# Padding tensors of the on-chip memory, so that the operands of the matmuls begin at multiples of 2 KB, and one of them 64 bytes behind

## The chip, the cores and the metric

The kernel runs on 1 core of one Trainium2 chip. The metric is the device time of one execution in microseconds (us). A core has TensorE (PE, the matmuls; the load of its stationary operand is listed apart as PEld), VectorE (DVE), ScalarE (ACT), GpSimd (POOL) and SyncE (SP, which here only issues DMAs). Operands lie in the on-chip memory, 128 partitions side by side; a tensor has the same byte offset in each partition, and this case is about that offset. TensorE writes to a memory of its own, the PSUM (here the tensors `H`, `YP`, `OP`).

## The reference

A channel attention over 6016 tokens of 256 channels, and then two feed-forward networks (FFNs), each from 256 to 2048 and back:

```python
qn = q / (np.linalg.norm(q, axis=1, keepdims=True) + 1e-06)     # q, k, v: (1, 6016, 256)
kn = k / (np.linalg.norm(k, axis=1, keepdims=True) + 1e-06)
s = kn.transpose(0, 2, 1) @ qn / tau                             # 256 x 256
a = softmax(s);  x = v @ a
h = x @ w_in1                                                    # 6016 x 2048
g = (a0 + a1*h + a2*h**2 + a3*h**3) / (1 + |b0|*|h| + |b1|*h**2 + 1e-6)
x = g @ w_out1                                                   # 6016 x 256
h = x @ w_in2                                                    # 6016 x 2048
g = h * clip(h + 3, 0, 6) / 6
out = g @ w_out2                                                 # 6016 x 256
```

## The kernel before, in words

**Stages.** `q` and `k` are loaded piece by piece (`qk`) and multiplied into a 256x256 sum in `OP` (line 471, in fp32). The softmax follows, and the attention matrix is folded into the first FFN's up-projection (`fold`, line 511), so that the rest of the kernel is two FFNs on `v`. The tokens are then worked off in 12 blocks: a first one of 384 tokens, and 11 of 512. The hidden 2048 are cut into 16 chunks of 128.

**Split products.** Each FFN product is made of three matmuls in fp32r (fp32 numbers that TensorE takes at one pass): both factors are split into a high and a low part (`_hi`, `_lo`), and `split_product` (lines 438 to 440) issues hi by hi, hi by lo and lo by hi into the same sum.

**The order on TensorE.** It is written out by hand in `step` (a loop over blocks `t`, with its chunks `j`). In each chunk TensorE issues four groups, 30 matmuls in all:

- `up2`: 6 matmuls of 512 columns. The moving operand is `yT_hi` or `yT_lo` (half c of the channels, 2 KB of each partition), the stationary one a slice of 128 columns (512 bytes) of `wu2_hi` or `wu2_lo`. The sum is in `H`.
- `down2`: 12 matmuls of 256 columns (lines 594, 596, 598). Here the gate is the stationary operand: four slices of 128 tokens (512 bytes) of `g2_hi` or `g2_lo`, and `wd2_hi` or `wd2_lo` moves (1 KB a chunk).
- `up1`: 6 matmuls of 512 columns. `vT_hi` or `vT_lo` moves, slices of `wf_hi`, `wf_lo` are stationary. The sum is in `H`.
- `down1`: 6 matmuls of 512 columns. The first FFN's gate, `g1_hi` or `g1_lo` (2 KB a chunk, four buffers), moves; slices of `wd1_hi`, `wd1_lo` are stationary. The sum is in `YP`.

The profile's names join some tensors: `g_hi` is `g1_hi` under `YP` and `g2_hi` under `OP`; `wd_hi`, `wu_hi` likewise.

Between the groups the gates are worked out from PSUM by ACT, DVE and POOL (lines 692 to 725, 889 to 937, 392 to 406), each held to TensorE by semaphores. `T`, `SQ`, `AB`, `Y` and `R` hold values on the way.

**Where the tensors lie.** They are placed one behind the other in the order in which the code makes them (`sb(name, shape, dt)`), each at the next free byte of the partition, rounded up to 32. There is some reserved space first, which ends 1152 bytes past a multiple of 2 KB. `wf`, `wd1`, `wd2`, `wu2` take 16 KB each, `vT` 4 KB each, so that all of these begin 1152 bytes past a multiple of 2 KB. Then come `ident`, `ones` (512 bytes each) and small tensors, then `v_blocks` (4 KB), `coef_row` and `o_tok` (4 KB); those small ones take 1344 bytes in all. From `o_tok` on (`w_raw_a` and `qk` in the attention's stage; `yT`, `R`, `g2`, `T`, `SQ`, `AB`, `Y`, `g1` in the same bytes later) everything begins 448 bytes past a multiple of 2 KB.

Of the kernel before, what the change touches and what calls it, by code (L numbers as in the profile page):

```python
# [20 lines left out]
fp32 = mybir.dt.float32  # L21
# [5 lines left out]
P = 128  # L27


def attention_ffn_ffn(nc, q, k, v, tau, w_in1, w_out1, a, b, w_in2, w_out2, out):  # L30
# [63 lines left out]
    with ctx:  # L94
        def sb(name, shape, dt, stack=ctx):
            return stack.enter_context(nc.sbuf_tensor(name, shape, dt))
# [2 lines left out]
            return ctx.enter_context(nc.semaphore(name))  # L99


        wf_hi, wf_lo = (sb(f"wf_{x}", [P, CT, F], f32r) for x in ("hi", "lo"))
        wd1_hi, wd2_hi = (sb(f"{x}_hi", [P, J, C], f32r) for x in ("wd1", "wd2"))
        wu2_hi = sb("wu2_hi", [P, CT, F], f32r)
# [15 lines left out]
        absb = sb("absb", [P, 2], fp32)  # L120
        root_b1 = sb("root_b1", [P, 1], fp32)[:]
        small = sb("small", [P, 48], fp32)

        v_blocks = sb("v_blocks", [P, CT, W], fp32)
        v_tok = v_blocks[:].rearrange("p h w -> p (h w)").rearrange("p (i c) -> p i c", c=C)
# [14 lines left out]

        yT_hi, yT_lo = (sb(f"yT_{x}", [P, CT, W], f32r) for x in ("hi", "lo"))
        R = sb("R", [P, 2, W], fp32)
        g2_hi, g2_lo = (sb(f"g2_{x}", [P, 4, W], f32r) for x in ("hi", "lo"))

        T = sb("T", [P, 2, W], fp32)
        SQ = sb("SQ", [P, 4, W], fp32)
# [67 lines left out]
        def back(blk, j, n):  # L214

            blk, j = blk + (j - n) // J, (j - n) % J
            return None if isinstance(blk, int) and blk < 0 else (blk, j)

        def wait_chunk(engine, semaphore, at):
            if at is not None:  # L220
                engine.wait_ge(semaphore, count(*at))
# [31 lines left out]
        def h2(blk, j):  # L253
            return H[:, 2 + j % 2, 0:width(blk)]
# [103 lines left out]
        def _(pool):  # L358
# [42 lines left out]
            def g2_split(blk, j):  # L401
                w = width(blk)
                if last_chunk(blk, j):
                    return
                wait_chunk(pool, g2_hi_done, (blk, j))
                nc.gpsimd.tensor_tensor(g2_lo[:, j % 4, 0:w], R[:, j % 2, 0:w], g2_hi[:, j % 4, 0:w].bitcast(fp32),  # L406
                                        ALU.subtract).then_inc(g2_lo_done, 1)
# [213 lines left out]
        def _(act):  # L621
# [93 lines left out]
            def c1(blk, j):  # L715
                w = width(blk)
                wait_chunk(act, u2_done, (blk, j))
                wait_chunk(act, g2_lo_done, back(blk, j, 2))
                nc.scalar.activation(R[:, j % 2, 0:w], h2(blk, j), ACT.Relu, bias=3.0).then_inc(r_done, 1)  # L719

            def c2(blk, j):
                w = width(blk)
                wait_chunk(act, g2_done, (blk, j))
                wait_chunk(act, d2_done, back(blk, j, 4))
                nc.scalar.activation(g2_hi[:, j % 4, 0:w], R[:, j % 2, 0:w], ACT.Copy).then_inc(g2_hi_done, 1)  # L725

# [68 lines left out]
        def _(dve):  # L795
# [126 lines left out]
            def gate2(blk, j):  # L922
                w = width(blk)
                wait_chunk(dve, r_done, (blk, j))
                nc.vector.scalar_tensor_tensor(R[:, j % 2, 0:w], R[:, j % 2, 0:w], 6.0, h2(blk, j),  # L925
                                               ALU.min, ALU.mult).then_inc(g2_done, 1)
                if last_chunk(blk, j):
                    wait_chunk(dve, g2_hi_done, (blk, j))
                    wait_chunk(dve, d2_done, back(blk, j, 4))
                    nc.vector.tensor_tensor(g2_lo[:, j % 4, 0:w], R[:, j % 2, 0:w],  # L930
                                            g2_hi[:, j % 4, 0:w].bitcast(fp32), ALU.subtract).then_inc(last_lo_done, 1)
# [57 lines left out]
```

## Time and profile before

| | |
|---|---|
| median of 3 runs | 1139.7 us (1139.54 to 1140.29) |
| the profiled execution | 1139.15 us, of it 1137.3 us span |
| PE busy | 1112.0 us, 98% of the span, 6012 matmuls |
| PEld busy | 961.3 us, 85% |
| DVE, ACT, POOL busy | 890.6 us (78%), 879.3 us (77%), 781.5 us (69%) |
| granted clock of TensorE | 0.995 of full |
| waits of PE on others | the longest group 7.8 us |

The span is the time from the first to the last recorded instruction. A matmul's busy time is longer than its share of the engine: matmuls overlap, and the next one starts while the one before is still under way. The pace is read from the distance between starts.

### The profile page before, as it was taken

How to read it: one execution, taken by the hardware profiler on the slowest of the kernel's cores; microseconds unless marked ns; L12 is line 12 of the kernel's file. 1: busy time of each engine (PE TensorE's matmuls, PEld its weight loads, DVE VectorE, ACT ScalarE, POOL GpSimd, SP SyncE). 2: the span in 40 equal slices, each digit the busy share in tenths (PEclk: the TensorE clock that was granted, in tenths of full speed). 3: DMA queues.
4: the chain of work that ended last, by engine and by line, in shares of the span. 5: the costliest groups of instructions: out<-in, count | busy, mean ns of one | idle time of the engine just before them, and what ended most of it. 6: DMA issues, size and time to landing. Idle time of an engine off the chain costs nothing.

```text
span 1137.3 us, 17913 instructions
## 1 busy us (share of the span) xinstructions
PE 1112.0 (98%) x6012; PEld 961.3 (85%) x6012; DVE 890.6 (78%) x1264; ACT 879.3 (77%) x1479; POOL 781.5 (69%) x625
## 2 busy tenths in 40 slices
PE   9988799999999999999999999999999999999998
PEld 8877588888888888888888888888888888888887
DVE  6699999887887887887887787787787787787722
ACT  6698888877877877877787787787787787787643
POOL 0278888776776776676676676677677677666643
PEclk9999899999999999999999999999999999999999
DMA  9931010010010010010010010010001000000000
GB/s 343 305 116 20 1 19 1 15 19 2 20 19 1 20 19 2 2 36 1 1 38 1 2 38 1 1 31 8 2 19 19 1 20 1 1 20 1 1 19 19
DMA packets 65729, 34.21 MB, mean 30 GB/s; under 512 B 47718, under 2 KB 58982, under 8 KB 65638
## 3 DMA queue, kind: packets, MB, share of 16 engines
q1 hardware_dynamic: 65072, 32.52, 10.1%
q8 instruction: 52, 0.85, 0.3%
q10 hardware_dynamic: 566, 0.52, 0.1%
q14 instruction: 39, 0.32, 0.1%
HBM read 26.87 MB, written 6.16 MB: 29 GB/s over the span
## 4 chain that ended last, share of the span: by engine, by line
PE 91%; DVE 5%; ACT 1%; issue 1%; DMA 0%; POOL 0%; SPq 0%; DVEq 0%; ACTq 0%
PE H L438 15%; PE H L440 14%; PE H L439 14%; PE OP L594 8%; PE OP L598 7%; PE OP L596 7%; PE YP L438 7%; PE YP L440 7%; PE YP L439 7%; PE OP L471 3%; DVE SQ L911 1%; DVE H L896 1%; DVE g_hi L904 1%; DVE T L889 1%; DMA qk<-in_k 0%
## 5 line engine op out<-in xcount | busy, mean ns | idle before, releaser
L392 POOL TENSOR_TENSOR SQ<-SQ,AB 128x512 f32<-128x512 f32 (+1 forms) x192 | 247.7, 1290 | 271.9 <-ACT SQ L694 271.6
L406 POOL TENSOR_TENSOR g_lo<-R,g_hi 128x512 fp32r<-128x512 f32 (+1 forms) x191 | 243.7, 1276 | 28.2 <-ACT g_hi L725 28.2
L398 POOL TENSOR_TENSOR g_lo<-SQ,Y 128x512 fp32r<-128x512 f32 (+1 forms) x192 | 244.2, 1272 | 6.2 <-DVE SQ L919 6.2
L692 ACT ACTIVATE AB<-H,absb 128x512 f32<-128x512 f32 (+1 forms) x192 | 130.6, 680 | 143.7 <-PE H L440 142.9
L594 PE MATMUL OP<-wd_hi,g_hi 128*128 128x256 f32 x748 | 208.1, 278 | 0.0
L598 PE MATMUL OP<-wd_hi,g_lo 128*128 128x256 f32 x748 | 207.8, 278 | 0.0
L596 PE MATMUL OP<-wd_lo,g_hi 128*128 128x256 f32 x748 | 207.8, 278 | 0.0
L889 DVE TENSOR_TENSOR T<-T,H 128x512 f32<-128x512 f32 (+1 forms) x192 | 129.4, 674 | 97.3 <-ACT T L700 97.3
L904 DVE SCALAR_TENSOR_TENSOR g_hi<-H,coef,Y 128x512 fp32r<-128x512 f32 (+1 forms) x192 | 141.7, 738 | 65.9 <-ACT Y L713 64.6
L438 PE MATMUL H<-vT_hi,wf_hi 128*128 128x512 f32 (+1 forms) x384 | 152.2, 396 | 13.6 <-DVE wf_lo L876 7.8
L911 DVE SCALAR_TENSOR_TENSOR SQ<-SQ,g_hi 128x512 f32<-128x512 f32 (+1 forms) x192 | 156.2, 814 | 6.6
L719 ACT ACTIVATE R<-H 128x512 f32<-128x512 f32 (+1 forms) x192 | 113.6, 591 | 57.1 <-PE H L440 56.4
L925 DVE SCALAR_TENSOR_TENSOR R<-R,H 128x512 f32<-128x512 f32 (+1 forms) x192 | 128.1, 667 | 36.9 <-ACT R L719 36.9
L438 PE MATMUL YP<-g_hi,wd_hi 128*128 128x512 f32 (+1 forms) x384 | 151.6, 395 | 4.9 <-POOL g_lo L398 3.3
L439 PE MATMUL H<-vT_lo,wf_hi 128*128 128x512 f32 (+1 forms) x384 | 150.8, 393 | 0.0
L438 PE MATMUL H<-yT_hi,wu_hi 128*128 128x512 f32 (+1 forms) x384 | 149.6, 390 | 0.8 <-issue 0.6
L440 PE MATMUL H<-yT_hi,wu_lo 128*128 128x512 f32 (+1 forms) x384 | 149.7, 390 | 0.0
L440 PE MATMUL YP<-g_hi,wd_lo 128*128 128x512 f32 (+1 forms) x384 | 149.1, 388 | 0.0
L439 PE MATMUL YP<-g_lo,wd_hi 128*128 128x512 f32 (+1 forms) x384 | 149.0, 388 | 0.0
L440 PE MATMUL H<-vT_hi,wf_lo 128*128 128x512 f32 (+1 forms) x384 | 148.7, 387 | 0.0
L896 DVE SCALAR_TENSOR_TENSOR H<-T,coef,H 128x512 f32<-128x512 f32 (+1 forms) x192 | 143.0, 745 | 6.8
L700 ACT ACTIVATE T<-H,coef 128x512 f32<-128x512 f32 (+1 forms) x192 | 147.8, 770 | 0.0
(98 smaller groups left out, 2208.1 us busy)
## 6 DMA issues: line engine op xcount, KB each, us to landing
qk<-in_q SPq DMA_DIRECT2D x22, 256.0 KB, 5.7
qk<-in_k SPq DMA_DIRECT2D x22, 256.0 KB, 6.9
v_blocks<-in_v SPq DMA_DIRECT2D x88, 64.0 KB, 2.3
out<-o_tok SPq DMA_DIRECT2D x10, 512.0 KB, 3.0
wd_raw<-in_moe_w_out SPq DMA_DIRECT2D x8, 512.0 KB, 9.3
w_raw_a<-in_moe_w_in SPq DMA_DIRECT2D x2, 1024.0 KB, 11.1
wu_raw<-in_moe_w_in SPq DMA_DIRECT2D x4, 512.0 KB, 6.3
qk<-in_q SPq DMA_DIRECT2D x3, 128.0 KB, 2.7
```

What stands on the lines that cost most here:

```text
L392: nc.gpsimd.tensor_tensor(SQ[:, j % 4, 0:w], SQ[:, j % 4, 0:w], AB[:, j % 2, 0:w], ALU.add)\
L398: nc.gpsimd.tensor_tensor(g1_lo[:, j % 4, 0:w], SQ[:, j % 4, 0:w], Y[:, j % 2, 0:w], ALU.mult)\
L406: nc.gpsimd.tensor_tensor(g2_lo[:, j % 4, 0:w], R[:, j % 2, 0:w], g2_hi[:, j % 4, 0:w].bitcast(fp32), ALU.subtract).then_inc(g2_lo_done, 1)
L438: nc.tensor.matmul(psum, w_hi, x_hi, start=first, stop=False)
L439: nc.tensor.matmul(psum, w_hi, x_lo, start=False, stop=False)
L440: return nc.tensor.matmul(psum, w_lo, x_hi, start=False, stop=last)
L594: nc.tensor.matmul(psum, g2_hi[:, j % 4, at], wd2_hi[:, j, :], start=first, stop=False, skip_group_check=True)
L596: nc.tensor.matmul(psum, g2_hi[:, j % 4, at], wd2_lo[:, j, :], start=False, stop=False, skip_group_check=True)
L598: done = nc.tensor.matmul(psum, g2_lo[:, j % 4, at], wd2_hi[:, j, :], start=False, stop=last, skip_group_check=True)
L896: nc.vector.scalar_tensor_tensor(h, T[:, j % 2, 0:w], A1, h, ALU.add, ALU.mult).then_inc(t3_done, 1)
L904: nc.vector.scalar_tensor_tensor(g1_hi[:, j % 4, 0:w], h1(blk, j), A0, Y[:, j % 2, 0:w], ALU.add, ALU.mult).then_inc(g1_hi_done, 1)
L911: nc.vector.scalar_tensor_tensor(SQ[:, j % 4, 0:w], SQ[:, j % 4, 0:w], Q_CONST, g1_hi[:, j % 4, 0:w].bitcast(fp32), ALU.add, ALU.mult).the ...
```

## The change

Four tensors are made that nothing reads or writes. They push what is made behind them to other offsets; no instruction is added, removed or moved in the order.

```diff
+        sb("up_to_2_kb", [P, 224], fp32)
         wf_hi, wf_lo = (sb(f"wf_{x}", [P, CT, F], f32r) for x in ("hi", "lo"))
...
         small = sb("small", [P, 48], fp32)
+        sb("up_to_4_kb", [P, 176], fp32)
 
         v_blocks = sb("v_blocks", [P, CT, W], fp32)
...
         R = sb("R", [P, 2, W], fp32)
+        sb("g2_offset", [P, 16], fp32)
         g2_hi, g2_lo = (sb(f"g2_{x}", [P, 4, W], f32r) for x in ("hi", "lo"))
+        sb("up_to_next_2_kb", [P, 496], fp32)
 
         T = sb("T", [P, 2, W], fp32)
```

The pads take 896, 704, 64 and 1984 bytes of each partition, 3648 in all. After it `wf`, `wd1`, `wd2`, `wu2` and `vT` begin at a multiple of 2 KB (1152 + 896 = 2048), `o_tok`, `w_raw_a`, `qk`, `yT` and `R` too (448 + 896 + 704 = 2048), `g2_hi` and `g2_lo` 64 bytes behind one, and `T`, `SQ`, `AB`, `Y`, `g1` at one again.

## Rows read from the trace of the kernel before

**Rows 1.** The page: busy time by engine, and busy tenths of 40 slices.
```profile
PE 1112.0 (98%) x6012; PEld 961.3 (85%) x6012; DVE 890.6 (78%) x1264; ACT 879.3 (77%) x1479; POOL 781.5 (69%) x625
PE   9988799999999999999999999999999999999998
PEclk9999899999999999999999999999999999999999
```
**Rows 2.** Waits of PE: who waited for whom, total us, times, longest.
```profile
PE H L438 <- DVE wf_lo L876: 7.8, 7, 2.3
PE H L438 <- DVE SQ L919: 5.7, 2, 5.1
```
**Rows 3.** Stretches: length, then busy us (instructions) by engine, clock, DMA, GB/s.
```profile
0.00:60.00 60.00, 56.45 (x271) 48.74 (x272) 39.03 (x55) 41.62 (x56) 11.86 (x13) 1.00 0.98 325
60.00:150.00 90.00, 72.75 (x353) 63.60 (x352) 84.20 (x135) 77.56 (x150) 73.97 (x65) 0.94 0.11 31
150.00:1137.00 987.00, 982.78 (x5392) 849.00 (x5391) 767.42 (x1076) 760.11 (x1275) 695.67 (x549) 1.00 0.05 12
300.00:1070.00 770.00, 769.41 (x4170) 661.31 (x4169) 617.20 (x866) 606.93 (x1014) 549.78 (x433) 1.00 0.05 12
```
**Rows 4.** PE in order of time, one chunk: start us, length us, matmul.
```profile
499.89 0.39 PE L438 MATMUL H<-yT_hi,wu_hi 128*128 128x512 f32 x1
...
501.04 0.40 PE L440 MATMUL H<-yT_hi,wu_lo 128*128 128x512 f32 x1
501.27 0.28 PE L594 MATMUL OP<-wd_hi,g_hi 128*128 128x256 f32 x1
...
501.97 0.28 PE L594 MATMUL OP<-wd_hi,g_hi 128*128 128x256 f32 x1
...
502.31 0.28 PE L594 MATMUL OP<-wd_hi,g_hi 128*128 128x256 f32 x1
...
502.65 0.40 PE L438 MATMUL H<-vT_hi,wf_hi 128*128 128x512 f32 x1
...
504.04 0.40 PE L438 MATMUL YP<-g_hi,wd_hi 128*128 128x512 f32 x1
...
504.74 0.39 PE L438 MATMUL YP<-g_hi,wd_hi 128*128 128x512 f32 x1
...
505.43 0.39 PE L438 MATMUL H<-yT_hi,wu_hi 128*128 128x512 f32 x1
```
**Rows 5.** PE in order of time, the last block (up2 and down2 alone).
```profile
1100.31 0.39 PE L438 MATMUL H<-yT_hi,wu_hi 128*128 128x512 f32 x1
...
1101.68 0.28 PE L594 MATMUL OP<-wd_hi,g_hi 128*128 128x256 f32 x1
```
**Rows 6.** The chain that ended last, in the attention: start, us, what.
```profile
22.98 20.72 PE OP L471 x96
```
**Rows 7.** PE and PEld groups of 300 to 1070 us: busy us, mean ns.
```profile
L439 PE MATMUL H<-vT_lo,wf_hi 128*128 128x512 f32 x278 | 109.9, 395 | 0.0
L440 PE MATMUL H<-yT_hi,wu_lo 128*128 128x512 f32 x278 | 109.7, 395 | 0.0
L440 PE MATMUL H<-vT_hi,wf_lo 128*128 128x512 f32 x278 | 108.2, 389 | 0.0
L439 PE MATMUL H<-yT_lo,wu_hi 128*128 128x512 f32 x278 | 107.9, 388 | 0.0
L439 PEld LDWEIGHTS H<-vT_lo,wf_hi 128*128 128x128 f32 x278 | 52.2, 188 | 5.6
```
**Rows 8.** The costliest DVE group, 128x512, whole span.
```profile
L911 DVE SCALAR_TENSOR_TENSOR SQ<-SQ,g_hi 128x512 f32<-128x512 f32 x176 | 143.1, 813 | 6.1
```

## The prediction

> **What bounds the kernel now.** I read the busy times first. PE is busy 98% of the span, at full clock, while DVE, ACT and POOL stand at 78, 77 and 69% [rows 1]. That alone proves little, because overlapping matmuls flatter PE, so the second look is at its waits: the two longest groups are 7.8 and 5.7 us in 1137.3 [rows 2], and both belong to the first stretch. The third is the table of stretches. From 60 to 150 us PE is busy 72.75 of 90 us, and DVE 84.20: there, while the fold and the first block run, DVE sets the pace. From 150 us on PE is busy 982.78 of 987 us, and from 300 to 1070 us 769.41 of 770, against 617.20 for DVE [rows 3]. So for 987 us nothing but the rate at which TensorE takes matmuls matters, and a change that touches no instruction can act on the time through that rate alone.
>
> **That rate.** The stretch of 770 us holds 4170 matmuls, and a chunk has 30, so it holds 139 chunks, 770 / 139 = 5.540 us each [rows 3]. One chunk in order of time splits it [rows 4]: `up2` from 499.89 to 501.27 is 1.38 us for 6 matmuls, 230 ns each; `down2` from 501.27 to 502.65 is 1.38 us for 12, 115 ns each; `up1` to 504.04 and `down1` to 505.43 are 1.39 us each, 232 ns a matmul. The sum is 5.54 us. Within the groups the pace isn't even. The second half of `down2`, 501.97 to 502.65, has 6 matmuls in 0.68 us, 113 ns each, against 117 ns in its first half [rows 4]. In the last block, where `up2` and `down2` alternate alone, the 6 long matmuls from 1100.31 to 1101.68 take 1.37 us, 228.3 ns each [rows 5].
>
> What could these be at best? In the attention 96 fp32 matmuls take 20.72 us, 215.8 ns each [rows 6]; they have 256 columns and evidently take two passes a column, so that they are as long as 512 columns of one pass. A long FFN matmul takes 230 to 232, 14 to 16 ns more. In a chunk 18 x 15 = 270 ns, and over the span some 50 us, are lost against the attention's pace, in a place where no engine waits. The excess differs between groups that are built alike: the matmuls with `vT_lo` moving are recorded with a mean of 395 ns and those with `yT_lo` with 388, `yT_hi` over `wu_lo` with 395 and `vT_hi` over `wf_lo` with 389 [rows 7]. `up1` and `up2` have the same instructions, the same sizes and the same sum tensor; they differ in the offsets of their operands and in the group ahead. So offsets may well matter at the level of 7 ns in a matmul (3%), and that is the only door this change has.
>
> The Trainium skill speaks against it. The page "SBUF — State Buffer", section "Who interferes with whom", gives TensorE two independent read ports, for the moving operand and for the weights, and says that it waits for nobody; "Operand start alignment" there calls the start address a matter of what is legal, not of speed. The page "TensorE: Matmul & The Clock Gate", section "Back-to-back issue gap", has N/2.4 + 2.5 ns, which is 215.8 ns for 512 columns. By this rule the sum of the change would be nothing. The attention's 215.8 ns agree with it [rows 6]; the FFNs' 230 to 232 ns don't [rows 4], so something acts there that the rule doesn't hold.
>
> **The change part by part.** No instruction goes or comes, no wait changes, and every wait is on the same semaphore as before.
>
> 1. *`wf`, `wd1`, `wd2`, `wu2`, `vT` from 1152 bytes past a multiple of 2 KB to 0; `yT`, `g1`, `w_raw_a`, `qk` from 448 to 0.* Two things change: the place in a 2 KB row, and the place of moving against stationary operand. The first I price low: slices of the gate `g2` begin at 448, 960, 1472 and 1984 bytes, so only the fourth crosses a multiple of 2 KB, and the third and fourth slices' matmuls from 501.97 to 502.31 and from 502.31 to 502.65 take 0.34 us each [rows 4]. A crossing costs nothing there. The second is the candidate: now `up1` has moving and stationary operands at like offsets, `up2` and `down1` at unlike ones (448 against 1152), `down2` likewise, and the reads of each matmul run beside the load of the next one's weights, so that at a change of group the relation changes too. The slow first halves of `down2` (117 against 113) stand just behind such a change.
> 2. *`g2` 64 bytes behind.* It acts on the weight loads of `down2`, and on the last matmul of `up2`, beside which the first of these loads runs. That one is the slowest of its group: 501.04 to 501.27, recorded with 0.40 us against 0.39 for the first [rows 4]; there both offsets are 448 today, thus alike.
> 3. *`T`, `SQ`, `AB`, `Y`, `R`, `v_blocks`, `o_tok`.* Reads and writes of DVE, ACT, POOL and the DMAs move. The nearest price is the costliest DVE instruction, 813 ns [rows 8]; if alignment took or gave 2% of 84.20 us of DVE in the stretch that DVE sets [rows 3], it would be 1.7 us either way. From 150 us on PE's bound covers it: DVE would have to grow by 770 / 617.20, 25%, before it showed. I take 0.
>
> **The sum.** For the unknown new pace I take the settled one that the trace already has: 228.3 ns for the long matmuls [rows 5] and 113.3 for the short ones [rows 4], since after the change all groups but `down2` share one relation of offsets, and `down2` avoids the equal one. A chunk is then 18 x 228.3 + 12 x 113.3 = 4109 + 1360 = 5469 ns, 71 less than 5540. Chunks in the stretch that PE sets: 987 / 5.54 = 178. The gain is 178 x 0.071 = 12.6 us. The profiled execution took 1139.15 us; less 12.6 that is 1126.6, and as it lies 0.55 us under the median of the runs, the forecast is 1127 us. The bounds of this term: at best the long ones come to the attention's 215.8 ns and the short stay, 18 x 215.8 + 1360 = 5244 ns, 296 less, -52.7 us; at worst every long one takes 240 ns (the slowest matmul of `up2` is recorded with 0.40 us where the first has 0.39, so 10 ns over the mean of 230) and every short one 117 [rows 4]: 4320 + 1404 = 5724 ns, 184 more, +32.8 us. I stay near the settled pace because it is the one that the same instructions already show.
>
> **The rivals.**
>
> *A. The full loss goes.* If the 15 ns are reads of moving and stationary operand that collide because of their starts, and like starts end that, the time is 1139.7 - 52.7 = 1087 us. For it: the attention's matmuls, with `qk` as both operands and thus like starts, have no excess [rows 6]. Against it: `up1` has like starts already and is no faster than the others [rows 4]; the attention reads only half as many columns in that time. DVE would then need 617.20 / 139 = 4.44 us of a chunk of 5.24, so it would not take over. Chance 12%.
>
> *B. Nothing, the change doesn't do what it says for the time.* The excess belongs to the matmuls of one pass a column and the order of groups, not to starts: the uncrossed and the crossing slice are alike, and the four groups lie within 0.01 us although their offsets differ [rows 4]. Time 1139.7 us. This is also where the rule of the Trainium skill's page "SBUF — State Buffer", section "Who interferes with whom", leads: reads that never wait for each other can't be helped by other starts. Chance 17%.
>
> *C. Slower: the like start is the dear one.* `up1`, alike today, shows 395 ns for `vT_lo` where `up2`, unlike, shows 388 for `yT_lo` [rows 7], and the slowest matmul of `up2` is the one beside which an alike load runs. If 12 long ones of `up2` and `down1` each take on 3 to 4 ns, half of that difference, it is 12 x 3.5 = 42 ns a chunk and 7.5 us in all: 1147 us. It decides from the point where what the gate's 64 bytes give back (at most 12 x 2 ns in `down2`) is less than that. Chance 23%.
>
> **How the numbers follow.** The forecast, faster by about 1%, has 48%, A 12%, B 17%, C 23%. A difference of 0.2% (2.3 us) is about what can be told from none. Faster: 48 + 12 = 60%; within 0.2%: 17%; slower: 23%. The likeliest case's own range is 1112 to 1137. The range for 8 in 10 reaches up into C, to 1149, and down between forecast and A, to 1100, leaving out most of A and the far end of C.
>
> **What would show it.** In the profile after, 139 chunks' worth of matmuls (4170) should take some 760 us in place of 770 in the middle stretch; the short ones should start 113 ns apart from the first on, the long ones 228. `yT_lo` and `vT_lo` matmuls should show the same mean. If `down2` alone changes, the 64 bytes are what acts; if the three long groups change alike, the common start. PE's busy share and waits should stay as they are. I am wrong if the distance between starts is unchanged (B), or if the long ones stand at 232 or more (C); and if the time moves while the pace of the middle stretch doesn't, the cause is in the first 150 us and part 3 was priced too low.

## The result, and the profile after

The kernel after takes 1136.69 us (median of 8 runs, 1136.19 to 1137.52) against 1139.64 us for the kernel before in the same comparison. The ratio is 0.9974, with a 95% interval of [0.9963, 0.9985]: faster by 0.26%, some 3 us. The forecast was 12.6 us. In the experiments below, one execution of the kernel before (1502 us) and one of x1 (2244 us) stand far from all others of their kernel, and the ratios leave them out.

The page of the kernel after, and its stretches (length, then busy us and instructions of PE, PEld, DVE, ACT, POOL, then clock, DMA share and GB/s), answer to [rows 1] and [rows 3]:

```profile
PE 1111.2 (98%) x6012; PEld 968.4 (85%) x6012; DVE 889.9 (78%) x1264; ACT 878.8 (77%) x1479; POOL 781.0 (69%) x625
```

```profile
0.00:60.00 60.00, 56.78 (x269) 48.95 (x270) 38.61 (x55) 41.46 (x55) 11.46 (x13) 1.00 0.95 316
60.00:150.00 90.00, 73.29 (x352) 64.02 (x351) 84.24 (x135) 77.48 (x151) 73.94 (x64) 0.94 0.13 37
300.00:1070.00 770.00, 769.24 (x4178) 667.73 (x4178) 617.59 (x868) 608.10 (x1017) 550.59 (x434) 1.00 0.05 12
```

Nothing but the pace has moved. PE is as busy as before, DVE takes 84.24 us of the second stretch against 84.20, and the two longest waits of PE are again 7.8 and 5.7 us:

```profile
PE H L444 <- DVE wf_lo L882: 7.8, 7, 2.3
PE H L444 <- DVE SQ L925: 5.7, 2, 5.1
```

In the same 770 us PE starts 4178 matmuls in place of 4170, so that a chunk takes 770 / (4178 / 30) = 5.529 us, 0.011 less (a rough count, since a few matmuls are missing from a trace). One chunk in order of time (start, length in us) shows where; it answers to [rows 4], with line 444 for 438 and 600 for 594:

```profile
505.06 0.39 PE L444 MATMUL H<-yT_hi,wu_hi 128*128 128x512 f32 x1
...
506.42 0.28 PE L600 MATMUL OP<-wd_hi,g_hi 128*128 128x256 f32 x1
...
507.12 0.28 PE L600 MATMUL OP<-wd_hi,g_hi 128*128 128x256 f32 x1
...
507.83 0.40 PE L444 MATMUL H<-vT_hi,wf_hi 128*128 128x512 f32 x1
...
509.22 0.39 PE L444 MATMUL YP<-g_hi,wd_hi 128*128 128x512 f32 x1
...
510.58 0.39 PE L444 MATMUL H<-yT_hi,wu_hi 128*128 128x512 f32 x1
```

`up2` has gone from 1.38 to 1.36 us and `down1` from 1.39 to 1.36; `up1` stays at 1.39; and `down2` has gone up, from 1.38 to 1.41. Its second half, 507.12 to 507.83, takes 0.71 us, 118 ns a matmul, where it took 113. The groups of 300 to 1070 us (busy us, mean ns) say it over all chunks and answer to [rows 7]:

```profile
L600 PE MATMUL OP<-wd_hi,g_hi 128*128 128x256 f32 x557 | 156.5, 281 | 0.0
L445 PE MATMUL H<-vT_lo,wf_hi 128*128 128x512 f32 x278 | 109.9, 395 | 0.0
L445 PE MATMUL H<-yT_lo,wu_hi 128*128 128x512 f32 x280 | 108.9, 389 | 0.0
L446 PE MATMUL H<-yT_hi,wu_lo 128*128 128x512 f32 x280 | 108.8, 389 | 0.0
L446 PE MATMUL YP<-g_hi,wd_lo 128*128 128x512 f32 x279 | 108.5, 389 | 0.0
```

All forms of `up2` and `down1` are now at 389 ns (390 for one), where `up2` over `wu_lo` stood at 395. A matmul's recorded length is its distance to the next start plus some 162 ns, so 389 is a start every 227 ns and 395 one every 233. `vT_lo` stays at 395.

### The profile page after: what moved, and what is told of

Read it like the earlier page. It is cut to its first block, busy times and chain, and to the rows that moved or that the text cites. A ratio compares the mean times of both kernels' runs of the same rounds, so it can differ in the third digit from the quotient of the medians.

```text
span 1135.7 us, 17913 instructions
## 1 busy us (share of the span) xinstructions
PE 1111.2 (98%) x6012; PEld 968.4 (85%) x6012; DVE 889.9 (78%) x1264; ACT 878.8 (77%) x1479; POOL 781.0 (69%) x625
## 4 chain that ended last, share of the span: by engine, by line
PE 91%; DVE 5%; ACT 1%; issue 1%; DMA 0%; POOL 0%; SPq 0%; DVEq 0%; ACTq 0%
PE H L444 15%; PE H L445 14%; PE H L446 14%; PE OP L604 8%; PE OP L600 8%; PE OP L602 8%; PE YP L445 7%; PE YP L446 7%; PE YP L444 7%; PE OP L477 3%; DVE SQ L917 1%; DVE H L902 1%; DVE g_hi L910 1%; DVE T L895 1%; DMA qk<-in_k 0%
## 5 line engine op out<-in xcount | busy, mean ns | idle before, releaser
L602 PEld LDWEIGHTS OP<-wd_lo,g_hi 128*128 128x128 f32 x748 | 142.7, 191 | 6.5
```

Source lines behind the costliest of these rows:

```text
L602: nc.tensor.matmul(psum, g2_hi[:, j % 4, at], wd2_lo[:, j, :], start=False, stop=False, skip_group_check=True)
```

## The experiments

All of them move tensors and nothing else. I give an offset as a distance: the start of the stationary operand less that of the moving one, counted within 256 bytes (why 256, x7 and x8 show). In the trace the first weights of a group are loaded beside the last matmul of the group ahead, so each change of group has a distance too. The table has two of them: `g2` less `yT` at the entry to `down2`, and `wf` less `wd2` at its exit. The way into `down1` (`wd1` less `vT`) is 0 in all kernels. The way into `up2` (`wu2` less `g1`) is 192 in before and x1, 128 in x6, 64 in x7 and x8, and 0 in all the others. The table gives each group's time as the mean over the chunks of 300 to 1070 us, in ns, from the starts of all matmuls in the trace (a few with a wait behind them left out; each cell is rounded by itself). The last two columns are the chunk's difference to before times 178, the chunks in the stretch that PE sets, and the measured difference of the medians.

| kernel | distances up2, down2, up1, down1 | entry, exit | up2 | down2 | up1 | down1 | chunk | x 178, us | measured, us |
|---|---|---|---|---|---|---|---|---|---|
| before | 192, 64, 0, 192 | 0, 0 | 1380 | 1377 | 1387 | 1390 | 5534 | | |
| after | 0, 64, 0, 0 | 64, 0 | 1359 | 1413 | 1387 | 1360 | 5520 | -2.5 | -2.95 |
| x1 | as before | 0, 0 | 1380 | 1377 | 1387 | 1390 | 5534 | 0 | +0.1 |
| x2 | as after | 64, 0 | 1359 | 1413 | 1388 | 1360 | 5520 | -2.5 | -2.8 |
| x3 | 0, 0, 0, 0 | 0, 0 | 1360 | 1432 | 1388 | 1360 | 5540 | +1.1 | +1.2 |
| x4 | 0, 192, 0, 0 | 192, 0 | 1359 | 1411 | 1370 | 1360 | 5500 | -6.1 | -5.4 |
| x5 | 0, 64, 0, 0 | 64, 0 | 1359 | 1413 | 1388 | 1360 | 5520 | -2.5 | -3.3 |
| x6 | 192, 64, 0, 128 | 0, 0 | 1392 | 1377 | 1387 | 1392 | 5547 | +2.3 | +0.6 |
| x7 | 0, 0, 0, 64 | 0, 0 | 1380 | 1432 | 1388 | 1400 | 5600 | +11.7 | +11.1 |
| x8 | 128, 128, 0, 64 | 0, 0 | 1403 | 1423 | 1387 | 1400 | 5613 | +14.1 | +13.2 |
| x9 | 0, 64, 0, 0 | 0, 64 | 1360 | 1413 | 1360 | 1360 | 5493 | -7.3 | -7.8 |
| x10 | 192, 64, 0, 0 | 0, 0 | 1397 | 1377 | 1387 | 1360 | 5520 | -2.5 | -2.9 |
| x11 | 0, 32, 0, 0 | 32, 0 | 1368 | 1418 | 1395 | 1372 | 5553 | +3.6 | +3.8 |
| x12 | 192, 64, 0, 0 | 192, 64 | 1390 | 1410 | 1360 | 1360 | 5520 | -2.5 | -2.6 |
| x13 | 0, 192, 0, 0 | 0, 192 | 1360 | 1417 | 1392 | 1364 | 5533 | -0.2 | -0.3 |

The sum over a chunk accounts for the time of every one of them within 1.7 us (x6, one run), most within 0.6. x6, x7, x8 and x11 are one run each beside the kernel before.

**x1 and x2: the place in the row, or the distance?** x1 keeps the first pad alone, x2 all but the first:

```diff
 x1
+        sb("up_to_2_kb", [P, 224], fp32)
 x2
+        sb("up_to_4_kb", [P, 176], fp32)
+        sb("g2_offset", [P, 16], fp32)
+        sb("up_to_next_2_kb", [P, 496], fp32)
```

> Of the four pads only the first (896 bytes) stands: every tensor of the FFNs moves by the same amount, wf, wd1, wd2, wu2 and vT to a multiple of 2 KB, yT, g1, g2 and the rest from 448 to 1344 past one, so no offset of one operand against another changes. Theory R (what counts is where the stationary operand begins against the moving one): every group keeps its pace, up2 1.38, down2 1.38, up1 and down1 1.39 us a chunk (5.54), time as before, 1139.6 us within 1.5. Theory M (what counts is the place of an operand in its 2 KB row): up1 has both operands at multiples of 2 KB in the kernel after and is no faster there (1.39 us), but wd1 and wu2 as stationary operands would carry a part of what up2 and down1 gained (0.02 and 0.03 us of a chunk), time 1133 to 1137 us.

> The first pad is taken away and the other three stand: wf, wd1, wd2, wu2, vT, yT and g1 all begin 1152 bytes past a multiple of 2 KB, g2 1216 past one. No operand but for those is at a multiple of 2 KB, but the offsets against each other are those of the kernel after. Theory R: paces as after, up2 and down1 1.36 us, down2 1.41, up1 1.39, time 1136.7 us within 1.5. Theory M: paces as before, 1.38, 1.39, 1.38, 1.39, time 1139.6.

x1: 1139.83 us, ratio 1.0002 [0.9992, 1.0013]. x2: 1136.94 us, 0.9976 [0.9966, 0.9986]. The groups of 300 to 1070 us, first of x1 and then of x2:

```profile
L597 PE MATMUL OP<-wd_hi,g_hi 128*128 128x256 f32 x556 | 154.4, 278 | 0.0
L443 PE MATMUL H<-yT_hi,wu_lo 128*128 128x512 f32 x278 | 109.7, 395 | 0.0
```

```profile
L599 PE MATMUL OP<-wd_hi,g_hi 128*128 128x256 f32 x559 | 157.1, 281 | 0.0
L445 PE MATMUL H<-yT_hi,wu_lo 128*128 128x512 f32 x280 | 108.8, 389 | 0.0
```

x1 has `wf`, `wd1`, `wd2`, `wu2` and `vT` at a multiple of 2 KB, and its lengths are those of before. x2 has no FFN operand at one (1152 and 1216 bytes past), and its lengths are those of after. The multiple of 2 KB does nothing that can be told; the offsets against each other carry the whole change. Theory M falls and R stands.

**x3, x4, x5: where g2 begins.** In the kernel after `g2` is moved to 0, 192 and 320 bytes behind (x5 also makes its pads up to 512 bytes only, not 2 KB):

```diff
 x3
-        sb("g2_offset", [P, 16], fp32)
-        sb("up_to_next_2_kb", [P, 496], fp32)
 x4
-        sb("g2_offset", [P, 16], fp32)
-        sb("up_to_next_2_kb", [P, 496], fp32)
+        sb("g2_offset", [P, 48], fp32)
+        sb("up_to_next_2_kb", [P, 464], fp32)
 x5
-        sb("up_to_2_kb", [P, 224], fp32)
+        sb("up_to_2_kb", [P, 96], fp32)
-        sb("up_to_4_kb", [P, 176], fp32)
+        sb("up_to_4_kb", [P, 48], fp32)
-        sb("g2_offset", [P, 16], fp32)
-        sb("up_to_next_2_kb", [P, 496], fp32)
+        sb("g2_offset", [P, 80], fp32)
+        sb("up_to_next_2_kb", [P, 48], fp32)
```

> The third and fourth pad are taken away, so that g2 too begins at a multiple of 2 KB, with no offset against wd2. Theory R1 (like starts are the good relation for all): down2 goes from 1.41 us back to 1.36 or 1.38, 0.03 to 0.05 us a chunk or 5 to 9 us, time 1128 to 1132. Theory R2 (the 64 bytes are there because a like start is worse in down2, whose loads take as long as its matmuls): down2 over 1.41 us, time over 1137, up to 1145.

> g2 begins 192 bytes behind a multiple of 2 KB in place of 64, so that stationary against moving operand in down2 is at the distance it had in the kernel before, counted in 512 bytes (448 - 1152 is 192 less than a multiple of 512 above it: 1344 = 2 x 512 + 320 one way, 192 the other). Theory R with the sign counted from the moving to the stationary operand: 192 isn't the old distance of 320, and down2 lies anywhere from 1.36 to 1.42 us. If the distance counts without a sign, down2 is back at 1.38 us or under while up2 and down1 keep 1.36: 5.49 us a chunk, 7 us less than before by down2's part and 9 in all, time 1130. Theory M (place in the row alone): down2 as after, 1.41, time 1136.7.

> All operands of matmuls begin at a multiple of 512 bytes (no longer of 2 KB: wf 1536 past one, yT 1024, g1 1536), but g2 begins 320 bytes behind one: the distance from the moving wd2 to the stationary g2 that the kernel before has (448 - 1152 = -704, which is 320 on from a multiple of 512). Theory R (the pace hangs on the distance from moving to stationary operand, counted within 512 bytes): up2 and down1 1.36 us as in the kernel after, down2 1.38 as before, up1 1.37 to 1.39: 5.48 to 5.49 us a chunk, 0.05 less than before, time 1130 to 1131 us. If 2 KB is what counts and not 512 bytes: up2 and down1 over 1.36 us and time over 1133.

x3: 1140.92 us, ratio 1.0012 [1.0003, 1.0022], slower than before. x4: 1134.32, 0.9951 [0.9933, 0.9969]. x5: 1136.95, 0.9973 [0.9962, 0.9984]. Their `down2` rows, one kernel a fence:

```profile
L598 PE MATMUL OP<-wd_hi,g_hi 128*128 128x256 f32 x556 | 156.7, 282 | 0.0
L600 PE MATMUL OP<-wd_lo,g_hi 128*128 128x256 f32 x556 | 157.4, 283 | 0.0
```

```profile
L600 PE MATMUL OP<-wd_hi,g_hi 128*128 128x256 f32 x560 | 156.3, 279 | 0.0
L444 PE MATMUL H<-vT_hi,wf_hi 128*128 128x512 f32 x278 | 109.0, 392 | 0.0
```

```profile
L600 PE MATMUL OP<-wd_hi,g_hi 128*128 128x256 f32 x559 | 157.2, 281 | 0.0
```

With `g2` at a like start `down2` is slower than 64 bytes behind (R2 holds): the 64 bytes are worth 19 ns a chunk there. x4 is 2.4 us faster than after, but not for the reason that I expected: `down2` has gained 2 ns a chunk, and `up1`, the group behind it, 17 (392 in place of 395 ns). x5 failed: `down2` has the distance of before, 320 within 512 bytes, and still 281 ns, not 278. So the distance alone doesn't set `down2`'s pace (x5 was forecast at 1130 to 1131 us).

**x6, x7, x8: other distances, one run each.** On the pads of x5, `yT` is moved on by 64, 256 and 384 bytes, `g1` by 128, 448 and 192, and `g2` begins at 320, 256 and 384; here x7:

```diff
+        sb("yt_offset", [P, 64], fp32)
         yT_hi, yT_lo = (sb(f"yT_{x}", [P, CT, W], f32r) for x in ("hi", "lo"))
         R = sb("R", [P, 2, W], fp32)
         g2_hi, g2_lo = (sb(f"g2_{x}", [P, 4, W], f32r) for x in ("hi", "lo"))
+        sb("up_to_next_2_kb", [P, 64], fp32)
...
+        sb("g1_offset", [P, 112], fp32)
         g1_hi, g1_lo = (sb(f"g1_{x}", [P, 4, W], f32r) for x in ("hi", "lo"))
```

> A look at other distances, stationary less moving within 512 bytes: up1 0, up2 448 (yT 64 behind), down1 384 (g1 128 behind), down2 320. Theory R: up2 and down1 leave 1.36 us a group, where 0 is the best long distance seen and 192 gives 1.37 to 1.38; down2 stays at 1.38. If a distance of 64 or more already frees the long matmuls of all collisions, these groups come down towards the attention's pace, 6 x 0.216 = 1.30 us. If long groups don't mind the distance beyond 'like or unlike', both show 1.38.

> Distances: up1 0, up2 256 (yT 256 behind), down1 64 (g1 448 behind), down2 256 (g2 256 behind). As for the look before: up2 and down1 between 1.30 and 1.40 us; down2 between 1.36 (113 ns a matmul) and 1.42, 1.38 if it is a half of 512 that matters, since 320 is near it.

> Distances: up1 0, up2 128 (yT 384 behind), down1 320 (g1 192 behind), down2 384 (g2 384 behind). Up2 and down1 between 1.30 and 1.40 us. Down2: at 0 it shows 1.43 us, at 64 and 192 1.41, at 320 1.38; if it falls steadily with the distance, 384 gives 1.37 or less, if 320 is a best place, 1.39 or more.

x6: 1140.79 us. x7: 1151.29. x8: 1153.4. None of the long distances comes near the attention's pace, and a steady 226.7 ns a matmul is seen at 0 alone. A distance of 0 isn't enough for it: `up2` in x7 has 0 too, but `g1` ahead of it lies 64 off, and it stands at 1380, like `up2` of before at 192. The three forecasts of 1.30 to 1.40 us for the long groups held but for `up2` in x8 (1.403); `down2` in x7 came out at 1.43, above its range of 1.36 to 1.42. The `down1` rows of x7 and of x8:

```profile
L445 PE MATMUL YP<-g_hi,wd_hi 128*128 128x512 f32 x276 | 108.8, 394 | 0.0
L603 PE MATMUL OP<-wd_lo,g_hi 128*128 128x256 f32 x548 | 155.1, 283 | 0.0
```

```profile
L445 PE MATMUL YP<-g_hi,wd_hi 128*128 128x512 f32 x274 | 108.0, 394 | 0.0
```

`g1` is 448 bytes behind in x7 and 192 in x8, which differ by 256, and both have 394 ns and 1400 a group. `g2` at 256 in x7 gives the 283 ns and the 1432 of x3, where it is at 0. So 256 bytes are the period, and x5's 320 was the 64 of the kernel after. But before has 64 too, and so does x6, whose `down2` is back at 1377: 64 goes with 118 ns in one kernel and with 113 in another. What differs is how the group is entered.

**x9, x10, x12: the entry.** All three stand on x5's first two pads. x9 moves `wd2` 192 bytes behind and puts `g2` at 0; x10 moves `yT` and, with it, `g2` to 64; x12 has x9's `wd2` and `yT` at 64, and a pad of 448 bytes that puts `g2` back to 0:

```diff
 x9, x12 (the same around wd2_raw and wd2_lo)
         wd1_hi = sb("wd1_hi", [P, J, C], f32r)
+        sb("wd2_hi_offset", [P, 48], fp32)
         wd2_hi = sb("wd2_hi", [P, J, C], f32r)
+        sb("wd2_hi_next", [P, 16], fp32)
 x10, x12
+        sb("yt_offset", [P, 16], fp32)
         yT_hi, yT_lo = (sb(f"yT_{x}", [P, CT, W], f32r) for x in ("hi", "lo"))
```

> wd2_hi and wd2_lo begin 192 bytes behind a multiple of 256, g2, yT and all other operands at one. So the stationary g2 is 64 on from the moving wd2 (counted within 256 bytes), as in the kernels before and after, and g2 begins like the yT that moves when its first slice is loaded, as in the kernel before and not in the one after. Theory E (down2's pace at a distance of 64 hangs on how it is entered: from a matmul whose moving operand begins like g2 it falls to 113 ns, otherwise it stays at 118): down2 1.38 us, with up2 1.36 to 1.37, up1 1.37 to 1.39, down1 1.36: 5.48 to 5.50 us a chunk, time 1129 to 1133 us. Theory D (the distance alone, and the 113 ns of before came from something else): down2 1.41 us, 5.53 a chunk, time 1137.

> Of the kernel after yT alone is moved on, to 64 bytes behind a multiple of 256, where g2 is too (wf, wd1, wd2, wu2, vT, g1 stay at multiples of 512). up2 has then the distance of before (192 within 256 bytes), down2 keeps its 64, and down2 is entered from a moving operand that begins like g2. Theory E: down2 1.38 us in place of 1.41 although neither g2 nor wd2 has moved; up2 1.38 to 1.39 as before; up1 1.39, down1 1.36: 5.51 us a chunk, time 1134 to 1136. Theory D: down2 1.41, up2 1.38: 5.55, time 1140.

> wd2 192 bytes behind a multiple of 256 and yT 64 behind, all else (wf, wd1, wu2, vT, g1, g2) at one. Up2 has the distance of the kernel before (192), down2 its 64, but g2 does not begin like the yT that moves when its first slice is loaded. Theory P (what up2 at a distance of 192 leaves behind sets down2's pace): down2 1.38 us, 113 ns in its second half. Theory E (both are wanted, the uneven up2 and the like start at the entry): down2 1.41 us, 118 ns throughout. Up2 1.38 to 1.40 either way, down1 1.36, up1 1.36 if it is the step from wd2 to wf at a distance of 64 that spares it its slow start. Time by P 1133 to 1136 us, by E 1138 to 1142.

x9: 1131.99 us, ratio 0.9929 [0.9912, 0.9947]. x10: 1136.87, 0.9973 [0.9963, 0.9984]. x12: 1137.14, 0.9979 [0.9969, 0.9988]. The `down2` rows of x10, x9 and x12, and for x9 also that of `up1`:

```profile
L600 PE MATMUL OP<-wd_hi,g_hi 128*128 128x256 f32 x556 | 154.3, 278 | 0.0
```

```profile
300.00:1070.00 770.00, 769.59 (x4205) 670.87 (x4204) 621.72 (x872) 610.26 (x1020) 553.49 (x437) 1.00 0.05 12
L607 PE MATMUL OP<-wd_hi,g_hi 128*128 128x256 f32 x563 | 158.3, 281 | 0.0
L452 PE MATMUL H<-vT_lo,wf_hi 128*128 128x512 f32 x278 | 108.2, 389 | 0.0
```

```profile
L609 PE MATMUL OP<-wd_hi,g_hi 128*128 128x256 f32 x559 | 156.8, 280 | 0.0
```

In x10 `g2` and `wd2` are as far apart as in the kernel after, `yT` alone has changed its place against both `wu2` and `g2`, and `down2` is back at 278 ns. x9 has the like start at the entry but an even `up2` (distance 0): 281. x12 has the uneven `up2` (192) but not the like start: 280 (its second half is at 118 ns). So in the middle stretch `down2` settles at 113 ns only where both are there (before, x1, x6, x10), as theory E said in x12; P and E as I had put it ahead of x9, with the like start alone, don't describe it. The forecasts of the time did worse: x12 lies between those of P and E, and x10 0.9 us above its own. The pair leaves a rival, too: x9 and x12 have moved `wd2`, so their exit differs from x10's as well.

Nor are the two conditions a rule for a single group. In the last block of the kernel before, where `up2` and `down2` alternate alone and the operands lie as ever, the first three `down2` run at 118 ns to their end, and the twelve behind them come to 113 (the sixteenth has another order of matmuls). Here is one of each, its second half and the start behind it:

```profile
1091.20 0.28 PE L594 MATMUL OP<-wd_hi,g_hi 128*128 128x256 f32 x1
...
1091.90 0.40 PE L438 MATMUL H<-yT_hi,wu_hi 128*128 128x512 f32 x1
```

```profile
1102.39 0.28 PE L594 MATMUL OP<-wd_hi,g_hi 128*128 128x256 f32 x1
...
1103.07 0.39 PE L438 MATMUL H<-yT_hi,wu_hi 128*128 128x512 f32 x1
```

The first takes 0.70 us for 6 matmuls, the second 0.68, with the same offsets. The other way round, in the kernel after, where `g2` and `yT` start unlike, the first `down2` of the last block, behind an `up2` that had to wait for `yT`, comes to 113 ns (its second half is 0.68 us), and the next one is back at 118:

```profile
1086.35 0.28 PE L600 MATMUL OP<-wd_hi,g_hi 128*128 128x256 f32 x1
...
1087.03 0.40 PE L444 MATMUL H<-yT_hi,wu_hi 128*128 128x512 f32 x1
```

x12 and x9 have such single groups too (at 1090.56 and at 1080.67 us). So the offsets decide at which pace the repeated chunk settles. What a single group does hangs also on what ran ahead of it, and neither the two conditions nor the place of `wd2` forbids 113 ns.

x9 is nevertheless the fastest of all, by a thing that I had not aimed at: its 1131.99 us lie within theory E's 1129 to 1133, although `down2` did not fall. Its `up1` runs at 389 ns, 1360 a group, like the other two. In order of time, around that exit:

```profile
505.32 0.28 PE L607 MATMUL OP<-wd_hi,g_hi 128*128 128x256 f32 x1
...
505.68 0.39 PE L451 MATMUL H<-vT_hi,wf_hi 128*128 128x512 f32 x1
...
507.04 0.39 PE L451 MATMUL YP<-g_hi,wd_hi 128*128 128x512 f32 x1
```

**x11 and x13: half the step, and the exit.** x11 puts `g2` 32 bytes behind; x13 is x9 with `wd2` 64 bytes behind in place of 192 (the pad behind it grows by as much):

```diff
 x11
-        sb("g2_offset", [P, 80], fp32)
-        sb("up_to_next_2_kb", [P, 48], fp32)
+        sb("g2_offset", [P, 8], fp32)
+        sb("up_to_next_2_kb", [P, 120], fp32)
 x13
-        sb("wd2_hi_offset", [P, 48], fp32)
+        sb("wd2_hi_offset", [P, 16], fp32)
```

> As the kernel after, but g2 begins 32 bytes behind a multiple of 256 in place of 64. If what collides is a unit of 64 bytes or more, 32 is still in the unit of a like start and down2 shows the 120 ns a matmul of the look with g2 at 0 (1.43 us), time about 1141. If the unit is 32 bytes or less, it shows 118 or another pace, and time is 1137 or under.

> As the kernel with wd2 192 behind, but wd2 begins 64 bytes behind a multiple of 256 and g2 at one: down2's distance is 192 in place of 64. By the looks so far down2 shows 1.41 us at either (x4 at 192, x9 at 64), the long groups 1.36 each, and the time is that of x9, 1132 us within 2. If the way out of down2 matters (load of wf 192 on from the moving wd2, in place of 64), up1 alone is slower, up to 1.39, and the time up to 1137.

x11: 1143.57 us, one run; `down2` at 1418 is neither the 1432 of 0 nor the 1413 of 64, so 32 bytes already make a difference in this one run, and the other groups suffer too (`up1` 1395). The expectation of 1137 us or under for a unit of 32 bytes or less was wrong. x13: 1139.45 us, 0.9998 [0.9989, 1.0008], above the 1137 that I had as its upper end. Its `down2`, at 192, and its `down1` are 4 ns each over x9's; the other 32 of the 40 ns that a chunk loses are in `up1`:

```profile
L451 PE MATMUL H<-vT_hi,wf_hi 128*128 128x512 f32 x278 | 111.1, 400 | 0.0
```

`up1` is 1392 there and 1360 in x9, with its own operands in the same places. So its pace is set by what is ahead of it: at an exit of 64 it is 1360 (x9, x12), at 192 1392, at 0 1387 in most kernels. The exit isn't all of it, for at 0 it is also 1370 in x4 and 1395 in x11, where `down2` itself has another distance.

## Why the prediction was wrong in size

The sign, the forecast's place (the rate of TensorE alone, no wait, no other engine) and the range were right; the size was a quarter. By its own steps:

- *What bounds.* Right. From 0 to 150 us nothing moved that can be told (DVE 84.24 us against 84.20), so part 3's price of 0 holds.
- *The long matmuls, 18 x 228.3 = 4109 ns a chunk.* The table has 1359 + 1387 + 1360 = 4106. The sum was right by luck in its parts: `up2` and `down1` fell under the settled pace, to 226.7 ns a matmul, and `up1` didn't move, since none of its distances changed. I had written that `up1` is alike today and no faster, and did not draw the conclusion that it would stay.
- *The short matmuls, 12 x 113.3 = 1360 ns.* This is the step that failed. They rose from 1377 to 1413. The term was off by 53 ns a chunk, 178 x 0.053 = 9.4 of the 12.6 us. Another 7 ns a chunk (1.2 us) were never there to be won: the 5540 that I started from hold the waits at the changes of block, and the groups by themselves add up to 5533. With the 3 ns by which the long matmuls beat their term, 71 - 53 - 7 + 3 = 14 ns a chunk or 2.5 us are left, and 2.95 were measured. I had taken the 113 ns of the second half as what `down2` comes to when it is left alone, and its slower first half as the price of the entry. The runs show the reverse for the middle stretch: `down2` settles at 113 ns behind an uneven `up2` and a like start (x10), and behind an even `up2` it runs at 118 from its first matmul to its last (x9, x5). Moving `yT` against `wu2` and `g2` took the 113 ns away; why it does stays open.
- *`down2` avoids the equal relation by the 64 bytes.* It does, but by these runs this gave nothing: counted within 256 bytes, `g2` lies 64 from `wd2` in the kernel before as well.
- *A crossing of a multiple of 2 KB costs nothing, the place in the row nothing.* The second is shown by x1 and x2; in both of them the second slice of `g2` crosses the multiple of 2 KB and not the fourth, and no pace changes.
- *Rival A, the whole excess goes.* Out: no distance tried brings the long matmuls of a group under 226.7 ns on average, 11 over the attention's 215.8 [rows 6].
- *Rival B, nothing, and the rule of the Trainium skill ("SBUF — State Buffer", "Who interferes with whom", that TensorE's two read ports are independent and it waits for nobody).* The traces disagree: the same matmuls run at 227 to 234 ns on average over a group as the distance changes (1359 in after to 1403 in x8), and x7 is 11 us slower than before with no instruction changed.
- *Rival C, a like start is dear.* Wrong for the long ones, where 0 gives the lowest group times of 0, 64, 128 and 192. Right for `down2` (x3, 120 ns): I had allowed at most 24 ns a chunk for the 64 bytes, and they are worth 19 against a like start. It pointed to the last matmul of `up2`. That one takes 236 ns in before and x10, 229 in x12, where the start is unlike, and 227 in x9, where it is like and `up2` even; so the like start alone doesn't make it slow.

That the reads of the moving operand and of the next weights get into each other's way in banks of the memory, and keep a phase from one matmul to the next, would fit much of this, but it is argued only. No run here separates it from another cause with the same period. Why 0 goes with the lowest times where the moving operand has 512 columns and with the highest where it has 256 stays open, too.

## What to carry to other kernels

When TensorE is busy all the time and waits for nobody, read the distance between starts, group by group, and look for groups of the same form at another pace: the offsets of operands against each other, within 256 bytes, are worth -0.7% (x9) to +1.2% (x8) of this kernel's time. Here not alignment but distance counted, and a group's pace moved with the operands of the group ahead too (`up1` from x9 to x13), so a pad that helps one group has to be priced in its neighbours. A pace that a trace shows in half of a group may be paid for by the other half or by the group ahead, and should not be taken as what is left when everything is even.

## What the runs showed of the hardware that I had not expected

- The pace is a fixed pattern, not a mean over chance: in the middle of the kernel before, the six starts of `up2` lie 232, 226, 229, 232, 226 and 236 ns apart in nearly every chunk, within 1 ns; in the kernel after 227, 227, 226, 227, 227 and 226.
- It hangs on the group ahead. In the last block of the kernel after, where `up2` stands behind `down2` and not behind `down1`, `up2` settles within 1 ns at the pattern that `up1` has elsewhere (233, 236, 229, 232, 231, 226), with its own operands where they were.
- It has a memory beyond the offsets: the same `down2` of the kernel before runs at 118 and at 113 ns in one block, as shown above.
- Offsets that differ by 256 bytes give the same times (x3 and x7, x7 and x8, x5 and after), and 32 bytes already make a difference (x11, one run).
- The fastest layout found, x9, is 7.8 us (0.7%) faster than before and some 4.7 us faster than after; the intervals of their ratios, [0.9912, 0.9947] and [0.9963, 0.9985], don't touch.
